# Threshold counts of the first expert stage: four columns of tokens in one product, then a mask, a folding product and a sum

## The reference

```python
for idx in order:                       # order = argsort of -logits
    tok, e = idx // E, idx % E
    if assigned[tok] >= 0 or counts[e] >= cap:
        continue
    assigned[tok] = e
    counts[e] += 1
h = np.maximum(x[mask] @ w1[e], 0.0)    # mask: the tokens of expert e
out[mask] = h @ w2[e]
```

## Time and profile before

| what | value |
|---|---|
| median of the runs | 1414.02 us |
| the profiled execution, whole | 1399.81 us |
| its span, first to last instruction | 1398.0 us |
| TensorE (PE) busy | 1288.9 us, 92% |
| weight loads (PEld) busy | 1193.0 us, 85% |
| VectorE (DVE) busy | 753.0 us, 54% |
| GpSimd (POOL) busy | 565.0 us, 40% |
| ScalarE (ACT) busy | 325.5 us, 23% |
| mean granted TensorE clock | 0.926 |

### The profile page before, as it was taken

One profiled execution on the slowest core, in us unless ns is written; L12 is line 12 of the kernel. 1 busy time (PEld: TensorE's weight loads), 2 busy tenths in 40 slices (PEclk: granted clock), 3 DMA queues, 4 the chain that ended last, 5 costly groups with the idle time before them and its releaser, 6 DMA issues.

```text
span 1398.0 us, 31508 instructions
## 1 busy us (share of the span) xinstructions
PE 1288.9 (92%) x10842; PEld 1193.0 (85%) x10843; DVE 753.0 (54%) x1978; ACT 325.5 (23%) x788; POOL 565.0 (40%) x556
## 2 busy tenths in 40 slices
PE   5999898737999999999999995999999999999996
PEld 4757798625998998888998995999999999999996
DVE  2733788895767568875554454433343333333342
ACT  0103100012232323232333331222222222222221
POOL 2800002203647474746556552421444142444411
PEclk9999755557999999999999998999999999999998
DMA  9605542001122222222232212221223122232110
GB/s 347 229 2 174 181 152 92 32 31 34 65 66 65 72 69 69 71 65 72 69 102 79 80 53 74 69 75 45 68 73 105 41 75 73 72 103 73 45 42 20
DMA packets 70734, 116.25 MB, mean 83 GB/s; under 512 B 7784, under 2 KB 50545, under 8 KB 70640
## 3 DMA queue, kind: packets, MB, share of 16 engines
q1 hardware_dynamic: 46864, 72.36, 15.6%
q0 software_dynamic: 11808, 31.03, 6.8%
q10 hardware_dynamic: 11968, 11.63, 3.0%
HBM read 81.83 MB, written 34.45 MB: 83 GB/s over the span
## 4 chain that ended last, share of the span: by engine, by line
PE 72%; DVE 13%; issue 1%; DMA 1%; ACT 1%; POOL 0%; ACTq 0%; POOLq 0%; DVEq 0%; SPq 0%
PE bank L1048 22%; PE bank L1050 21%; PE bank L1049 21%; PE bank L954 3%; DVE arena L1562 2%; DVE hot_r L1668 2%; PE bank L1187 1%; PE bank L943 1%; PE bank L1060 1%; DVE hot_q L1669 1%; DVE hot_q L1667 1%; DVE opens L1628 1%; DVE hT_low L1831 0%; DVE xT_low L1824 0%; DVE arena L1612 0%
## 5 line engine op out<-in xcount | busy, mean ns | idle before, releaser
L1048 PE MATMUL bank<-weights_high,hT_high 128*128 (+1 forms) x1328 | 388.1, 292 | 0.0
L1050 PE MATMUL bank<-weights_high,hT_low 128*128 (+1 forms) x1328 | 378.9, 285 | 0.0
L1049 PE MATMUL bank<-weights_low,hT_high 128*128 (+1 forms) x1328 | 377.9, 285 | 0.0
L1048 PE MATMUL bank<-xT_high,weights_high 128*128 128x256 f32 (+1 forms) x1072 | 336.3, 314 | 6.4 <-DVE xT_low L1824 3.7
L1050 PE MATMUL bank<-xT_high,weights_low 128*128 128x256 f32 (+1 forms) x1072 | 332.9, 311 | 0.0
L1049 PE MATMUL bank<-xT_low,weights_high 128*128 128x256 f32 (+1 forms) x1072 | 332.0, 310 | 0.0
L1050 PEld LDWEIGHTS bank<-weights_high,hT_low 128*128 128x128 f32 x1328 | 250.7, 189 | 0.0
L1048 PEld LDWEIGHTS bank<-weights_high,hT_high 128*128 128x128 f32 x1328 | 250.4, 189 | 0.1
L1049 PEld LDWEIGHTS bank<-weights_low,hT_high 128*128 128x128 f32 x1328 | 250.1, 188 | 0.0
L1048 PEld LDWEIGHTS bank<-xT_high,weights_high 128*128 128x128 f32 x1072 | 205.1, 191 | 19.9 <-DVE xT_low L1824 4.5
L1050 PEld LDWEIGHTS bank<-xT_high,weights_low 128*128 128x128 f32 x1072 | 204.0, 190 | 11.6
(11 more groups left out here) (242 smaller groups left out, 1473.0 us busy)
## 6 DMA issues: line engine op xcount, KB each, us to landing
arena<-middle ACTq DMA_DIRECT2D x44, 258.0 KB
spectrum<-arena SPq DMA_DIRECT2D x39, 256.0 KB, 2.2
arena<-in_w2a_t SPq DMA_DIRECT2D x8, 1024.0 KB, 5.4
raw<-in_w1a SPq DMA_DIRECT2D x8, 1024.0 KB, 5.1
raw<-in_w2a SPq DMA_DIRECT2D x8, 1024.0 KB, 5.6
raw<-in_w1b SPq DMA_DIRECT2D x8, 1024.0 KB, 5.1
raw<-in_w2b SPq DMA_DIRECT2D x8, 1024.0 KB, 5.7
arena<-in_x SPq DMA_DIRECT2D x4, 768.0 KB, 4.5
```

Of the source, the lines that this page charges most:

```text
L1048: pe.matmul(out_, a[0], b[0], start=start, stop=False)
L1049: pe.matmul(out_, a[0], b[1], start=False, stop=False)
L1050: return pe.matmul(out_, a[1], b[0], start=False, stop=stop)
```

## The change

The 8 counts inside the expert stage are done in another way; the 20 counts ahead of it stay as they are.

- `above_quads` in place of `above_count`: four columns of tokens are one product, with a stationary operand of 128x128 (4 columns x 32 probes) and a moving one of 128x32 (4 columns x 8 experts). The result is 128x32 in bank 7, of which only the four diagonal blocks of 32x8 are wanted. The pieces become 24, 28 and 26 columns, so that there are 6 + 7 + 7 = 20 products (one of them of two columns).
- `spread_quads` on VectorE, where `mark` stood: the 128x32 result times a mask `own` that keeps the diagonal blocks, written to `spread`.
- `fold_quads` on TensorE behind part f = 7 of `hidden`, ahead of `places`: a float32 product of the 128x32 constant `fold` with `spread`, which adds the four partition groups: 32x32 in bank 7.
- `mark_folded` on VectorE behind `h_out` 7, ahead of `placed`: a sum over the four column blocks into `counts`, and the comparison with the places left, which sets `s_pass`.
- The waits of bank 7 go with them: the count names the masking as its reader (`s_spread`), the folding product names `s_pass`.

```diff
-LATER_CHUNKS = (0, 26, 52, N // P)
+LATER_CHUNKS = (0, 24, 52, N // P)
+QUAD = 4
...
+    put("own", p // PROBES == np.arange(QUAD * E)[None, :] // E)
+    put("fold", p % PROBES == np.arange(PROBES)[None, :])
...
+        def quads_at():
+            return bank[7][:, 384:384 + QUAD * E]
+
+        def folded_at():
+            return bank[7][0:PROBES, 416:416 + QUAD * E]
...
@@ -947,12 +959,30 @@
 
             def above_count(ph, r):
 
-                to, pieces = count_at(ph), chunks(ph)
+                to, pieces = count_at(), chunks(ph)
                 for c in range(len(pieces) - 1):
                     pe.wait_ge(s_above, above_done(ph, r) + c + 1)
                     for j in range(pieces[c], pieces[c + 1]):
                         mm = pe.matmul(to, above[:, j, :], hot8[:, j, :], start=(j == 0), stop=(j == NT1 - 1))
                 mm.then_inc(s_above_ps, 1)
+
+            def above_quads(ph, r):
+
+                to, pieces = quads_at(), chunks(ph)
+                for c in range(len(pieces) - 1):
+                    pe.wait_ge(s_above, above_done(ph, r) + c + 1)
+                    j, odd = pieces[c], (pieces[c + 1] - pieces[c]) % QUAD
+                    while j < pieces[c + 1]:
+                        w = odd if j == pieces[c] and odd else QUAD
+                        mm = pe.matmul(to[0:w * PROBES, 0:w * E], above[:, j:j + w, :].rearrange("p j k -> p (j k)"),
+                                       hot8[:, j:j + w, :].rearrange("p j e -> p (j e)"), start=(j == 0), stop=(j + w == NT1))
+                        j += w
+                mm.then_inc(s_above_ps, 1)
+
+            def fold_quads(ph, r):
+
+                pe.wait_ge(s_spread, (ph - SERIAL) * ROUNDS + r + 1)
+                pe.matmul(folded_at(), cc("fold"), spread[:], start=True, stop=True).then_inc(s_folded, 1)
 
             def move(ph, r):
 
@@ -1033,12 +1063,16 @@
 
             def route_count(G, f):
 
+                if f == FCH - 1 and G in COMPARE_AT:
+                    ph, r = COMPARE_AT[G]
+                    route_read(s_pass, ph * ROUNDS + r + 1)
+                    fold_quads(ph, r)
                 if f != COUNT_BEHIND.get(G, 1):
                     return
                 if G in COMPARE_AT:
                     ph, r = COMPARE_AT[G]
-                    route_read(s_pass, ph * ROUNDS + r + 1)
-                    above_count(ph, r)
+                    route_read(s_spread, (ph - SERIAL) * ROUNDS + r + 1)
+                    above_quads(ph, r)
                 if G == FINAL_AT:
                     route_read(s_closed, E - SERIAL)
                     new_count(E - 1, hot8)
@@ -1565,7 +1599,18 @@
             def mark(ph, r):
 
                 dve.wait_ge(s_above_ps, ph * ROUNDS + r + 1)
-                dve.tensor_tensor(passes[:], count_at(ph), left_open[0:PROBES, :], ALU.is_ge).then_inc(s_pass, 1)
+                dve.tensor_tensor(passes[:], count_at(), left_open[0:PROBES, :], ALU.is_ge).then_inc(s_pass, 1)
+
+            def spread_quads(ph, r):
+
+                dve.wait_ge(s_above_ps, ph * ROUNDS + r + 1)
+                dve.tensor_tensor(spread[:], quads_at(), cc("own"), ALU.mult).then_inc(s_spread, 1)
+
+            def mark_folded(link, ph, r):
+
+                dve.wait_ge(s_folded, (ph - SERIAL) * ROUNDS + r + 1)
+                link(dve.tensor_reduce(counts[:], folded_at().rearrange("p (j e) -> p e j", e=E), AX.X, ALU.add))
+                dve.tensor_tensor(passes[:], counts[:], left_open[0:PROBES, :], ALU.is_ge).then_inc(s_pass, 1)
 
             def floors_at(r):
                 return (floors[(r + u) % 2][:] if r + u else floor[:] for u in range(2))
@@ -1810,9 +1855,14 @@
             def marking(G):
 
                 if G in COMPARE_AT:
-                    mark(*COMPARE_AT[G])
+                    spread_quads(*COMPARE_AT[G])
                 if G == FINAL_AT:
                     counted_new(on_limit.link, E - 1)
+
+            def folded(G):
+
+                if G in COMPARE_AT:
+                    mark_folded(on_limit.link, *COMPARE_AT[G])
 
             def stage1(m, fast):
 
@@ -1912,6 +1962,8 @@
                                     marking(e * NG + gi)
                             gated(e, gi)
                             h_out(*nxt, 7)
+                            if fast:
+                                folded(e * NG + gi)
                         else:
                             for part in range(4):
                                 routed(e, gi, part)
@@ -1932,6 +1984,7 @@
                 h_out(0, 0, f)
                 if f == MARK_BEHIND:
                     marking(-1)
+            folded(-1)
             for e in range(E):
                 expert(e, e % 2, e == E - 1)
```

More of the change, by code:

```diff
@@ L69 @@
 CHUNKS = (0, 24, 48, 68, N // P)
-LATER_CHUNKS = (0, 26, 52, N // P)
+LATER_CHUNKS = (0, 24, 52, N // P)
+QUAD = 4
+assert QUAD * PROBES == P
 DCH = D // P
@@ L120 @@
       ("sign", 1), ("lane", 1), ("lane2", 1), ("valid", TPE), ("beyond", TPE), ("span", G2 + 1),
-      ("fresh4", E * (1 + GT)), ("fresh2", E * 3), ("parts", PROBES * ROUNDS)]
+      ("fresh4", E * (1 + GT)), ("fresh2", E * 3), ("parts", PROBES * ROUNDS), ("own", QUAD * E), ("fold", PROBES)]
 COL = {}
@@ L336, in build_program @@
         alone = sb("alone", [P, E])
+        spread, counts = sb("spread", [P, QUAD * E]), sb("counts", [PROBES, E])
         id_f, order_i = sb("id_f", [P, 1]), sb("order_i", [P, E], I32)
@@ L400, in build_program @@
         s_order, s_limit = sem("s_order"), sem("s_limit")
+        s_spread, s_folded = sem("s_spread"), sem("s_folded")
         s_moved, s_closed, s_prefixed, s_added = (sem(n) for n in ("s_moved", "s_closed", "s_prefixed", "s_added"))
@@ L469, in above_done, with count_at @@
             return before + r * (len(chunks(ph)) - 1)
-        def count_at(ph):
-            return bank[0][0:PROBES, 0:E] if ph < SERIAL else bank[7][0:PROBES, 64:64 + E]
+        def count_at():
+            return bank[0][0:PROBES, 0:E]
+        def quads_at():
+            return bank[7][:, 384:384 + QUAD * E]
+        def folded_at():
+            return bank[7][0:PROBES, 416:416 + QUAD * E]
         def move_at(ph):
```

## The result

The changed kernel takes 1405.79 us, the median of five runs from 1404.85 to 1407.33 us; the kernel before took 1413.91 us beside it (five runs, 1411.46 to 1414.27). The ratio is 0.9950, with a 95% interval of 0.9939 to 0.9962: 8.1 us faster. The prediction said 2.8 us slower.

A forecast was written before the change was run, and what follows sets the result against it. TensorE's instruction stream was taken to set the pace. Shorter counts -10.1 us, added waits +12.8 and one fold +0.15 gave +2.8 us, added to the runs' 1414.0: 1416.8 us, range 1412 to 1425 (the case's own 1415.5 to 1421).

The forecast's parts named there:

- The step that failed: Whole kernel: the +2.8 us worked out on the profiled execution (1399.81 us) is added to the runs' median, 1414.0 us.
- the three signs: Changed kernel's profile: `places` right behind the folding product, 20 products over 1 us, or a changed clock would disprove the prediction.
- The count: Eight counts: 20 products at 30 ns take 0.60 instead of 2.04 us, saving 1.44 us each, 10.1 us over seven.
- Group 0 keeps nothing: Group 0: part 4 waits for VectorE's L1831 anyway, so the shorter count saves 0 there.
- The wait: Ahead of `places` in groups 0 to 6: TensorE waits for `mark_folded`, seven waits of 1.8 us, 12.8 us in all.
- the fold of group -1: Group -1: the folding product is on the path and adds 0.15 us; in seven groups the wait hides it.
- The ends of the range: Whole kernel: 26 ns a product, 0.65 us for the comparison, group 0 keeping 0.56 us give 1415.5 to 1421 us.
- Rival (a): Seven new waits: they let TensorE's clock fall; 1423.6 us with four falls, 1428.7 with all seven; chance 0.20.
- Rival (b): Eight old counts: they let the clock fall in undisturbed runs, 1.7 us each, and the change ends that; 1403.2 us; chance 0.12.
- Rival (c): New counts: wide loads aren't hidden, 97 ns a product, saving 0.7 instead of 10.1 us; 1426.2 us; chance 0.04.
- Rival (d): Groups 1 and 4: VectorE holds them as it does group 0, so their saving is lost; 1419.7 us; chance 0.09.

The follow-up runs named there:

- after_third: The changed kernel, unchanged, run once more on chip 9 beside the kernel before (1399.81 us): 1402.48 us, ratio 1.0025.
- early_fold_second: The same kernel as early_fold, run again on chip 9 beside the kernel before (1399.81 us): 1390.84 us, ratio 0.9944.
- early_fold: The changed kernel with the folding product one part of `hidden` earlier and `mark_folded` ahead of the last two evacuations: 1393.50 us, kernel before 1413.37 us.
- quads_at_2_5: early_fold with the wide count in groups 2 and 5 alone, the old count in the other six: 1395.55 us, ratio 0.9986 to the kernel before.
- narrow_third: early_fold with the old 78-product count in groups 2 and 5 alone, on chip 1: 1406.26 us, ratio 0.9959 to the kernel before.
- before_again: The kernel before, unchanged, with a new profile on chip 15: 1412.31 us, ratio 0.9994.
- after_again: The changed kernel, unchanged, run again on chip 15: 1405.50 us, ratio 0.9949 to the kernel before.

## Why the prediction was wrong

**The step that failed** is the last one: "The median of the runs is 14.2 us above that execution, for a reason that the trace doesn't show; I add the same 2.8 us to it". The sum was made for a clean execution, and was near for one: +2.8 us forecast, +2.7 us by the medians on chip 9 (+3.5 us by the ratio, with an interval from 2.1 to 4.9). The runs were late executions, in which the old counts of groups 2 and 5 cost 5.7 us more each. The wide count doesn't pay that, so there the sum needs a further term: 2.8 - 2 x 5.7 = -8.6 us against the -8.1 measured (-7.0 with the terms as measured, below). The 14.2 us were no constant offset but a cost of the very instructions that were being replaced. The notice was there: a gap of 1% between trace and runs, five times the change that was forecast. None of the three signs that the prediction named for being wrong came: they look at the changed kernel's trace alone, and what failed lay in the kernel before.

**Point by point, in the clean trace** (after_third). The end of group 0, all engines, and the count of group 2:

```profile
369.39 0.40 PE L1084 MATMUL bank<-xT_high,weights_low 128*128 128x512 f32 x1
...
369.72 0.25 PE L985 MATMUL bank<-spread,cst 128*32 128x32 f32 x2
...
370.47 0.68 DVE L1881 SCALAR_TENSOR_TENSOR hT_low<-bank,hT_high 128x512 fp32r<-128x512 f32 x1
371.07 0.17 DVE L1612 TENSOR_REDUCE counts<-bank 32x8 f32<-32x32 f32 x1
371.27 0.15 DVE L1613 TENSOR_TENSOR passes<-counts,left_open 32x8 bf16<-32x8 f32 x1
...
371.57 0.20 PE L1141 MATMUL bank<-kinds_in,tri_b 128*128 128x32 bf16 x1 [1.60 <-DVE passes L1613]
...
403.01 0.86 PE L977 MATMUL bank<-arena 128*128 128x32 bf16 x20
403.72 0.48 PE L1082 MATMUL bank<-xT_high,weights_high 128*128 128x512 f32 x1
```

- *The count.* 20 products take 0.71 us to the next large one, 36 ns each; forecast 30, from the earlier trace rows. The saving is 1.33 us, not 1.44. The term was 0.8 us too good over seven groups.
- *Group 0 keeps nothing.* Part 4 starts at 363.98 after an idle time of 0.44 us ended by L1881, as in the earlier trace rows. `places` of group 0 comes at 371.57, where the earlier trace rows have 371.63. The first says that the forecast is right: from the count's start to part 4 it is 5.27 us, before 5.17. That the second numbers agree is chance: the count of group 0 starts 2.10 us earlier (0.98 of it before the stage begins, 1.12 kept by group -1), and the wait of the next point uses that up.
- *The wait.* From where `places` could start (369.63, as 0.24 us follow the last large product's start) to where it does: 1.94 us, forecast 1.86. The distance to the evacuation's end is 1.44, as in the earlier trace rows; the two operations take 0.35 us from 371.07 to 371.42, and TensorE starts 0.15 us later, where the earlier trace rows had 0.06. L1613 takes 0.15 us and not L1880's 0.65. Seven idle times of 1.50 or 1.60 us, as named.
- *The sum of each group.* From `places` to `places` the changed kernel takes 21.32 instead of 20.84 us (groups 0 to 1), 21.19 instead of 20.63 (1 to 2), 31.80 instead of 31.26 (2 to 3): +0.5 to +0.6, where 1.86 - 1.44 made +0.4.
- *The agreement of the total is partly luck.* The terms as measured are -1.33 x 7 = -9.3 us for the counts, +13.4 for the waits (five of 1.94, two of 1.84) and some 0.3 for the fold of group -1 and the rest: +4.4 us. From the first changed count to the last `places` the clean traces say the same, 528.02 us against 523.54. That the whole executions are only 2.7 us apart comes from the stage's start (0.98 us earlier) and from what follows the last `places` (0.8 us shorter), where both kernels do the same.
- *Smaller slips of the working.* The ends of the range that it names (26 ns, 0.65 us, group 0's 0.56 us) add up to 1415.7 and 1420.0 us, not 1415.5 and 1421. And L1880 isn't slow merely beside a gather: in groups 1 and 4 of the kernel before it takes 0.20 us with one beside it.
- *Rival (a) is false.* At the seven waits the clock stays at 1.00, and the window from 340 to 540 us is at 0.99 as in the earlier trace rows.
- *Rival (b) had the side, the place and nearly the size* (1403.2 us; measured 1405.8), with a chance of 0.12. Its mechanism was another: the five unbroken counts of a late chip see no fall of the clock. Two counts are idle for 3.9 us each, and the fall of the clock comes with that, 1.8 us each: two events of 5.7 us, not eight of 1.7. The row that it was read from isn't of the old count's products alone either: between 175 and 200 us four counts take some 9.4 us, and float32 products of 16 columns (L943) most of the rest.
- *Rival (c) is false.* 36 ns a product is far from 97. The Trainium skill's rule (TensorE: Matmul & The Clock Gate, LDWEIGHTS), 1.2 columns a nanosecond, would make 107 ns of each load. The profile of the changed kernel records 95 to 107 ns for one load by itself, which is near it, but in the stream they follow each other at 36 ns, so that as a price per product the trace disagrees.
- *Rival (d)* isn't seen: groups 1 and 4 keep their saving, as their distances say.

**The price of the fold.** In early_fold_second the folding product lies in the stream, and `places` waits for nothing:

```profile
368.73 0.40 PE L1084 MATMUL bank<-xT_high,weights_low 128*128 128x512 f32 x1
369.06 0.25 PE L985 MATMUL bank<-spread,cst 128*32 128x32 f32 x2
...
369.24 0.50 PE L1082 MATMUL bank<-xT_high,weights_high 128*128 128x512 f32 x1
...
370.74 0.20 PE L1141 MATMUL bank<-kinds_in,tri_b 128*128 128x32 bf16 x1
```

It lengthens the step between two large products from 0.24 to 0.51 us, by 0.27 us (forecast 0.15 for a fold on the path). 7 x (1.94 - 0.27) = 11.7 us is what early_fold should gain over the changed kernel, and 12.0 (chip 15) and 11.6 us (chip 9) are measured.

**A better version.** early_fold beats both kernels on both kinds of chip: 1393.5 against 1413.4 and 1405.5 us on a late one, 1390.8 against 1399.8 and 1402.5 on a clean one. The wide count is worth having; its mark has to be off `places`' way.

**What stays open.** What makes a chip late: each chip was met once, so that chip and moment can't be told apart. How indirect stores hold up three engines there: the instruction supply, the release of one engine by another and the recording of the profile itself, which in late profiles lacks landing times, are rivals that no run separates. Whether it is the stores or the close row of them, since every late count had at least two. And quads_at_2_5 on a late chip wasn't seen, so that S rests on narrow_third and on the traces of before_again and after_again.

## What to carry to other kernels

When the profiled execution and the timed runs of one kernel differ by more than the change is expected to bring, the gap is the first thing to explain: it may be the cost of the very instructions that change. "<-issue" in the middle of a run of small products means that something holds up TensorE which the profile doesn't show; here fewer, wider products helped, though they save little in a clean trace, and so did moving the stores beside them. And a shared bank turns a new reader into a wait: name its reader where that reader has been done for long, one part of the work earlier if need be.

## What the runs showed of the hardware

Beside GpSimd's indirect stores other engines are held up on some chips. The old count is 156 instructions (78 loads, 78 products) in 2.04 us, 13 ns each; the new one 40 in 0.71 us. On three of the six chips of the experiments the old one breaks off, in groups 2 and 5 after some 45 products, when four indirect stores run beside it, and goes on at 4 to 5 products each 0.72 us; the new one was unbroken beside the same stores. ScalarE and VectorE start single instructions 1.3 to 1.7 us late beside four stores on such a chip. The Trainium skill (Runtime: NRT & Kernel Launch, Instruction fetch mechanics) says that the sequencer fetches its instructions ahead over a DMA queue of its own, and that this is hidden behind the rate at which they are issued. The trace agrees with the first half: it lists queues of kind "instruction" with packets of 8 and 16 KB. It doesn't contradict the second, since the late count of group 2 passes without such a packet.

The same program differs by 1% from chip to chip, 11.4 of 13.0 us of it by the two broken counts and the clock that falls in them: 1397.6 to 1399.8 us on three, 1412.3 to 1413.4 us on three others.

The clock doesn't fall behind an idle time of 1.6 us in any of the seven waits. It does in the count with 3.1 us of idle time in pieces, to 0.50 for nearly 7 us (405.9 to 412.7 us), beside what the earlier trace rows showed for 2.16 us.
